# W3 times the last weights, moved out of its own stage and into the heads of attention

## The reference

```
attn_out = softmax(mask(q @ k.T / 8)) @ v       # mask: query and key have the same 6 sign bits
x  = attn_out as 1536 x 512
h  = x @ moe_w_in                               # 512 x 2048
y  = (s * relu(h)**2 + b) @ moe_w_out           # 2048 x 512
out = ((y @ w1) * (y @ w2)) @ w3 @ w_out        # 512 x 1024 (twice), 1024 x 1024, 1024 x 512
```

## Time and profile before

| | us |
|---|---|
| median of 3 runs (lowest, highest) | 792.26 (791.89, 794.51) |
| the profiled execution | 792.57 |
| its span, first to last instruction | 790.8 |
| PE busy | 763.3 (97%) |
| DVE busy | 458.7 (58%) |
| ACT busy | 369.1 (47%) |
| POOL busy | 238.9 (30%) |

### The profile page before, as it was taken

The page is one execution under the profiler, slowest core; times in us unless marked ns, Lnnn a source line. Parts: engine busy times, 40 slices in busy tenths (PEclk is TensorE's granted clock), DMA queues, the critical chain, the costliest instruction groups (busy, mean ns, idle before and its releaser), DMA issues.

```text
span 790.8 us, 11231 instructions
## 1 busy us (share of the span) xinstructions
PE 763.3 (97%) x3680; PEld 624.4 (79%) x3680; DVE 458.7 (58%) x809; ACT 369.1 (47%) x686; POOL 238.9 (30%) x150
## 2 busy tenths in 40 slices
PE   3999999999989899999999999999999999999998
PEld 2788888788878688888888888888887888888886
DVE  4899999999979711376665566655584201210220
ACT  2889998898889932443223132331352111211211
POOL 3347655674565744652022020220211000000000
PEclk9999999999999999999999999999999999999999
DMA  5343344334522232241011010110010010001001
GB/s 151 80 118 77 94 98 98 75 93 96 125 86 64 66 114 82 80 158 53 1 54 34 20 53 0 53 28 26 11 44 0 1 40 14 1 15 39 0 0 53
DMA packets 17680, 45.37 MB, mean 57 GB/s; under 512 B 4946, under 2 KB 6994, under 8 KB 17650
## 3 DMA queue, kind: packets, MB, share of 16 engines
q1 hardware_dynamic: 17650, 44.99, 20.7%
HBM read 37.75 MB, written 3.19 MB: 52 GB/s over the span
## 4 chain that ended last, share of the span: by engine, by line
PE 82%; DVE 7%; ACT 4%; issue 4%; DMA 2%; SPq 0%; POOL 0%; DVEq 0%; ACTq 0%
PE psum L986 55%; PE psum L1073 8%; PE psum L940 6%; PE psum L927 5%; PE psum L916 3%; DVE top L745 3%; PE psum L910 2%; ACT prob L524 2%; ACT pt_hi L540 1%; DVE pt_lo L759 1%; DVE x_lo L863 1%; PE psum L901 1%; DMA stage<-in_w_out 1%; PE psum L898 1%; DVE qm L738 1%
## 5 line engine op out<-in xcount | busy, mean ns | idle before, releaser
L759 DVE TENSOR_TENSOR pt_lo<-psum,pt_hi 128x384 fp32r<-128x384 f32 x192 | 97.8, 549 | 11.8 <-ACT pt_hi L540 10.2
L524 ACT ACTIVATE prob<-psum,exp_at 128x768 f32<-128x768 f32 x96 | 96.3, 1003 | 11.6 <-DVE exp_at L752 11.3
L745 DVE TENSOR_REDUCE top<-psum 128x1 f32<-128x768 f32 x96 | 90.9, 946 | 4.3 <-PE psum L916 4.1
L540 ACT ACTIVATE pt_hi<-psum 128x384 fp32r<-128x384 f32 x192 | 84.2, 493 | 19.1 <-PE psum L927 17.7
L632 ACT ACTIVATE relu<-psum 128x512 f32<-128x512 f32 x48 | 28.5, 596 | 137.0 <-PE psum L986 137.0
L986 PE MATMUL psum<-x_hi,w_b 128*128 128x512 f32 (+1 forms) x288 | 90.6, 396 | 0.0
L986 PE MATMUL psum<-x_hi,w_c 128*128 128x512 f32 (+1 forms) x288 | 90.6, 396 | 0.0
L927 PE MATMUL psum<-ident,prob 128*128 128x128 f32 x576 | 83.5, 280 | 4.2 <-DVE pt_lo L759 3.9
L886 DVE TENSOR_TENSOR ab<-psum,a_sb 128x512 f32<-128x512 f32 x24 | 16.6, 691 | 121.3 <-ACT a_sb L682 121.3
L840 DVE SCALAR_TENSOR_TENSOR relu<-psum,relu 128x512 f32<-128x512 f32 x48 | 33.1, 689 | 88.0 <-ACT relu L632 82.9
L403 POOL TENSOR_TENSOR w_b<-stage,w_b 128x1024 fp32r<-128x1024 f32 x18 | 43.6, 2425 | 125.0 <-ACT w_b L551 124.2
(11 more groups left out here) (91 smaller groups left out, 1459.7 us busy)
## 6 DMA issues: line engine op xcount, KB each, us to landing
raw<-in_qk SPq DMA_DIRECT2D x30, 384.0 KB, 5.2
stage<-in_w_out SPq DMA_DIRECT2D x12, 512.0 KB, 3.3
stage<-in_w3t SPq DMA_DIRECT2D x8, 512.0 KB, 3.9
stage<-in_w_in SPq DMA_DIRECT2D x8, 512.0 KB, 3.3
stage<-in_w SPq DMA_DIRECT2D x8, 512.0 KB, 3.2
raw_v<-in_v SPq DMA_DIRECT2D x16, 192.0 KB, 2.8
qm<-both_hi SPq DMA_DIRECT2D x16, 192.0 KB, 2.7
r_sb<-r_rows SPq DMA_DIRECT2D x16, 192.0 KB, 5.4
```

The lines of the kernel that those rows point to most:

```text
L524: act.activation(prob[:, t % 3], score[t % 2], ACT.Exp, bias=exp_at[:, t % 2, 1:2], scale=exp_at[:, t % 2, 0:1], accum_out=rsum[:, (t // 6 ...
L540: act.activation(pt_hi[:, u % 2, 3 * part:3 * part + 3, (t % 3) * P:(t % 3 + 1) * P], turned[part].rearrange("p (j q) -> p j q", j=3), ACT ...
L745: dve.tensor_reduce(top[:, t % 2, 1:2], score[t % 2], AX.X, ALU.max, negate=True).then_inc(top_done, 1)
L759: dve.tensor_tensor(pt_lo[at], turned[part].rearrange("p (j q) -> p j q", j=3), pt_hi[at].bitcast(F32), ALU.subtract).then_inc(pt_lo_done, 1)
```

## The change

The 8 blocks of `wc` are cut in halves of 256 columns (`g` = 0 to 15). Halves 0 to 13 are computed in heads 2 to 15, one per head, 6 matmuls in each of the head's last four tiles, into bank 7 after the head's sign bits are read from it; the last block is computed whole after attention. ACT copies each half to `wc_raw`, unsplit, and it is split into `wc_hi` (ACT) and `wc_lo` (POOL instead of DVE) in the first steps of the first layer. To have the weights in time, the last weights are loaded and split in pair 0, one chunk of W3 in every pair, and chunk 12 (the first layer's first) in pair 7. `x_raw` becomes a full-size buffer that shares its place with `x_lo`, and `wc_raw` one with `wc_lo`. PE, ACT and POOL write the middle pairs out instead of looping; DVE keeps its loop.

SP, the order of the loads:

```diff
+            for w in range(2):
+                load_w(w, w, w_out2[:, w * WCH:(w + 1) * WCH])
+
+            def pair(pr, first=False, last=False):
                 for k in range(2):
...
+                    if first and k == 0:
+                        load_w(2, 0, w_out2[:, 2 * WCH:3 * WCH])
+                    if first and k == 1:
+                        load_w(W3, 0, w3t[0])
+                    if not first and k == 0:
+                        load_w(W3 + pr, pr % 2, w3t[pr])
+                    if last and k == 0:
+                        load_w(of_layer(0), 0, w_in[0])
                     if last and k == 1:
-                        load_w(W3 + 1, 1, w3t[1])
+                        load_w(of_layer(0) + 1, 1, w_out[0])
                     sums_out(h, k, pr)
...
+                    if first and k == 0:
+                        load_w(3, 1, w_out2[:, 3 * WCH:4 * WCH])
                     sums_in(h, k, pr)
```

POOL, in the pairs (in pair 0 `w_out2_low(0)` stands first, 1 behind `scale_q`, 2 behind `k_lo`, 3 behind `x_of(0)`), and behind attention:

```diff
+            def w3_low(i):
+                w_low(W3 + i, high(w_b, i % 2), low(w_b, i % 2), i % 2)
+                pool.wait_ge(w_lo_done, W3 + i + 1)
...
                 if last:
-                    w_out2_low(2)
-                    w_out2_low(3)
+                    w3_low(pr)
...
                     k_lo(2 * pr + 3, 1)
                     pool.wait_ge(k_lo_done, 2 * pr + 4)
+                    w3_low(pr)
+                else:
+                    w_low(of_layer(0), high(w_c, 0), low(w_c, 0), 0)
+                    pool.wait_ge(w_lo_done, of_layer(0) + 1)
...
-            with pool.Fori(1, FT // 2) as ip:
-                for k in range(2):
-                    w_low(2 * ip + k + W3, high(w_b, k), low(w_b, k), k)
...
-            first_layer_weights(of_layer(0), 0)
+            w_low(of_layer(0) + 1, high(w_c, 1), low(w_c, 1), 1)
             pool.wait_ge(w_lo_done, of_layer(0) + 2)
             pool.memset(y_acc[:, :, :], 0.0).then_inc(y_zero, 1)
...
             for k in range(4):
                 w_low(W12_A + k, high(w_a, k), low(w_a, k), k % 2)
+            for i in range(FT):
+                pool.wait_ge(wc_hi_done, i + 1)
+                pool.tensor_tensor(wc_lo[:, i], wc_raw[:, i], wc_hi[:, i].bitcast(F32),
+                                   ALU.subtract).then_inc(wc_lo_done, 1)
```

ACT, at the end of a tile, after attention, and in steps 2 and 3 of the first layer:

```diff
+            def wc_copy(g):
+
+                act.wait_ge(wc_mm_done, g + 1)
+                act.activation(wc_raw[:, g // 2, (g % 2) * FC:(g % 2 + 1) * FC], wc_ps,
+                               ACT.Copy).then_inc(wc_raw_done, 1)
...
+                    if first and t in (1, 2, 5, 8):
+                        w = (1, 2, 5, 8).index(t)
+                        w_high(w, w // 2 + 1, w % 2, high(w_a, w))
+                    if (first and t == 11) or (last and t == 2) or (not (first or last) and t == 8):
+                        w_high(W3 + pr, (W3 + pr) // 2 + 1, pr % 2, high(w_b, pr % 2))
+                    if last and t == 8:
+
+                        act.wait_ge(k_lo_done, HEADS)
+                        w_high(of_layer(0), of_layer(0) // 2 + 1, 0, high(w_c, 0))
+                    if t % 6 == 5 and not first:
+                        wc_copy(h - 2)
...
+            act.wait_ge(wc_mm_done, HEADS - 1)
+            act.activation(wc_raw[:, FT - 1], psum[:, 2, :], ACT.Copy).then_inc(wc_raw_done, 1)
...
+            w_high(of_layer(0) + 1, of_layer(0) // 2 + 1, 1, high(w_c, 1))
...
+                    if first and k in (2, 3):
+                        for i in range(4 * k - 8, 4 * k - 4):
+                            wc_high(i)
```

PE, between `scores` (or `dots`) and `weighted`, and after attention; on DVE the loop that made `wc_lo` is gone:

```diff
+            def fused_terms(i, cols):
+                k = i % 2
+                return [(w[k][:, j], o[:, j, cols]) for j in range(FT)
+                        for w, o in ((w3_hi, wo2_lo), (w3_lo, wo2_hi), (w3_hi, wo2_hi))]
+
+            def fused_part(g, part, bits):
+
+                if part == 0:
+                    pe.wait_ge(w_lo_done, W3 + g // 2 + 1)
+                    pe.wait_ge(bits_done, bits)
+                    after(pe, wc_raw_done, g)
+                terms = fused_terms(g // 2, slice((g % 2) * FC, (g % 2 + 1) * FC))
+                for i in range(6 * part, 6 * part + 6):
+                    mm = pe.matmul(wc_ps, terms[i][0], terms[i][1], start=(i == 0), stop=(i == len(terms) - 1))
+                if part == 3:
+                    mm.then_inc(wc_mm_done, 1)
...
+                            after(pe, wc_raw_done, h - 2)
...
+                    if not first and t % 6 > 1:
+                        fused_part(h - 2, t % 6 - 2, min(2 * h + 4, 2 * HEADS))
...
-            for k in range(2):
-                fused(k, k)
-            with pe.Fori(1, FT // 2) as ip:
-                for k in range(2):
-
-                    pe.wait_ge(wc_lo_done, 2 * ip + k - 1)
-                    fused(2 * ip + k, k)
-
+            pe.wait_ge(w_lo_done, W3 + FT)
+            product(2, fused_terms(FT - 1, slice(0, DM))).then_inc(wc_mm_done, 1)
```

More of the change, by code:

```diff
@@ L57, in attention_mlp @@
         w_b = sb("w_b", [P, 4 * WCH], FR)
+        with ExitStack() as before_split:
+            wc_raw = sb("wc_raw", [P, FT, DM], F32, before_split)
+        wc_lo = sb("wc_lo", [P, FT, DM], FR)
         with ExitStack() as a:
@@ L289, in rows_of_chunk @@
                 return w[bass.ds(c, 1)].rearrange("o p n -> (o p) n")
-            pair(0)
-            for pr in range(1, PAIRS - 2):
+            pair(0, first=True)
+            for pr in range(1, PAIRS - 1):
                 pair(pr)
-            for w in range(2):
-                load_w(w, w, w_out2[:, w * WCH:(w + 1) * WCH])
-            for k in range(2):
[L297 to L303, removed]
-            pair(PAIRS - 1, last=True)
-            with sp.Fori(1, FT // 2) as ip:
-                for k in range(2):
[L307 to L310, removed]
+            pair(PAIRS - 1, last=True)
+            load_w(of_layer(1), 0, w_in[1])
+            load_w(of_layer(1) + 1, 1, w_out[1])
             for k in range(4):
@@ L414, in w_out2_low, with pair @@
                 pool.wait_ge(w_lo_done, w + 1)
-            def pair(pr, first=False, last=False, before_last=False):
+            def w3_low(i):
+                w_low(W3 + i, high(w_b, i % 2), low(w_b, i % 2), i % 2)
+                pool.wait_ge(w_lo_done, W3 + i + 1)
+            def pair(pr, first=False, last=False):
+                if first:
+                    w_out2_low(0)
                 if not first:
@@ L427, in pair @@
                     pool.wait_ge(q_scaled, 2 * pr + 4)
+                if first:
+                    w_out2_low(1)
                 if not first:
@@ L438, in pair @@
                     pool.wait_ge(k_lo_done, 2 * pr + 3)
+                if first:
+                    w_out2_low(2)
                 if not first:
@@ L446, in pair @@
                 pool.wait_ge(x_done, 4 * pr + 1)
-                if before_last:
-                    w_out2_low(1)
-                if not (last or before_last):
+                if first:
+                    w_out2_low(3)
+                if 2 * pr + 4 < HEADS:
                     scale_q(pr + 2, 0)
@@ L465, in _ @@
             pair(0, first=True)
-            with pool.Fori(1, PAIRS - 2) as pr:
+            for pr in range(1, PAIRS - 1):
                 pair(pr)
-            pair(PAIRS - 2, before_last=True)
             pair(PAIRS - 1, last=True)
-            w_low(W3 + 1, high(w_b, 1), low(w_b, 1), 1)
-            pool.wait_ge(w_lo_done, W3 + 2)
             x_of(2 * HEADS - 2, 2, PAIRS - 1)
@@ L562, in _, with pair @@
             exps(1, 1, 0)
-            def pair(pr, first=False, before_last=False, last=False):
+            def pair(pr, first=False, last=False):
                 for t in range(12):
@@ L584, in pair @@
                         v_high(2 * pr + 1, pr, 1)
[L585 to L592, removed]
-                        w_high(W3 + k, 3, k, high(w_b, k))
+                    if first and t in (1, 2, 5, 8):
[8 more added lines that the diff above has]
+                        wc_copy(h - 2)
             pair(0, first=True)
-            with act.Fori(1, PAIRS - 2) as pr:
+            for pr in range(1, PAIRS - 1):
                 pair(pr)
-            pair(PAIRS - 2, before_last=True)
             pair(PAIRS - 1, last=True)
@@ L622, in first_layer_weights, with wc_high @@
                     w_high(w + k, count, k, high(layer_buf[par], k))
-            first_layer_weights(of_layer(0), of_layer(0) // 2 + 1, 0)
-            fused(FT - 1, 1)
+            def wc_high(i):
+                act.activation(wc_hi[:, i], wc_raw[:, i], ACT.Copy).then_inc(wc_hi_done, 1)
             def hidden(n, k):
@@ L976, in _ @@
             pair(0, first=True)
-            with pe.Fori(1, PAIRS - 1) as pr:
+            for pr in range(1, PAIRS - 1):
                 pair(pr)
@@ L1077, in _ @@
             pe.wait_ge(w_lo_done, W12_A + 4)
+            pe.wait_ge(wc_lo_done, FT)
             pe.wait_ge(y_lo_done, KT)
```

54 lines of the change are left out of this document (12 added, 42 removed).

## The result

| | before | after |
|---|---|---|
| median of the runs | 792.94 us (791.89 to 794.51, 6 runs) | 787.38 us (785.65 to 790.35, 6 runs) |
| profiled execution, its span | 792.57, 790.8 us | 785.65, 783.7 us |
| ratio after / before | | 0.9934 (0.9915 to 0.9952) |

The change makes the kernel faster by 5.6 us. The forecast was 782.0, a gain of 10.6 us: the direction is right and the time lies inside the range, but only half of the gain came. So the question for the experiments was where the other 5 us went.

The account below looks back on a forecast made before the run. PE was taken to bound both attention, where it is held up only 1.2 us per head, and the wc stage; +25.6 us in attention and -36.2 behind it gave -10.6 on 792.57, so 782.0 us, range 773 to 791.

Parts of the forecast that it names:

- pairs 1 to 5: Ten heads of attention, 17.7 us each with the added matmuls: 177.0 for 157.0, +20.0 us.
- pair 6: Attention: loads of the last weights leave the pair, removing ACT's 2.45 us wait; 35.4 for 35.55, -0.15 us.
- head 14: First head of the last pair: 15.89 us becomes 17.6, +1.7 us.
- head 15: Last head: PE waits in its last three tiles, only one of four parts falls before; +0.5 us (0 to 2.9).
- pair 0: Start of attention: five added chunk copies on ACT and a possibly late chunk, +3.5 us (zero to 7.7).
- behind attention: From attention's end to the first product of out_of_hidden(0): 54.8 becomes 18.6 us, -36.2, with PE waiting 1.5 for the clearing.
- The price of the added matmul: Attention: each added matmul of 256 columns costs PE 0.120 us, 24 per head cost 2.9 us.
- Rival 3: Attention: weight load of the short matmul shows, 0.175 us each, +17.2 us, 799; chance 0.08.
- a quarter of today's 1.2 us survive as jitter: Attention: PE's work of 17.4 us per head plus part of today's hold-up gives 17.7 us per head.
- Rival 1: Attention: gaps around dots and the loops' register waits shrink too, 17.1 us per head, -7.8, near 774; chance 0.15.
- Rival 2: Attention: uneven copies on ACT delay turn, 18.6 us per head, +11.7, near 794, no change; chance 0.12.
- rival 4: Attention: W3's chunks come late, about 4 us in each of seven pairs, 810 us; chance 0.04.

Follow-up runs that it names:

- everything in time: Kernel after with W3's last chunk loaded in pair 6, y_acc cleared first, chunk 2 issued earlier, w_out2_low(3) behind k_lo: 776.69 us, 0.9805 of before.
- the mended kernel: Kernel after with only the load of W3's last chunk moved from pair 7 to the second half of pair 6: 783.81 us, 0.9883 of before.
- both edits and the later copies in pair 0: Kernel after with W3's last chunk loaded in pair 6, y_acc cleared first, last weights' chunks 2 and 3 copied at tiles 7 and 9: 781.44 us.

## Why the forecast was right in direction and wrong in size

| term | forecast | measured in the profiled execution |
|---|---|---|
| pairs 1 to 5 | +20.0 | +16.9 (173.9 for 157.0) |
| pair 6 | -0.15 | -0.9 (34.67 for 35.55) |
| head 14 | +1.7 | +4.4 (20.33 for 15.89) |
| head 15 | +0.5 | +2.8 (23.68 for 20.88) |
| pair 0 | +3.5 | +5.0 (tile 12 at 53.85 for 48.81) |
| behind attention | -36.2 | -35.5 (19.3 for 54.8) |
| sum | -10.6 | -7.2 (span -7.1, profiled time -6.9) |

- **The price of the added matmul held.** 0.120 us taken, 0.72 / 6 = 0.120 found. Rival 3 is out. The Trainium skill's rule in "TensorE: Matmul & The Clock Gate", section "The mechanism" (loads overlap matmuls only when the row groups differ), by which it would be an estimated 0.21 us as the prediction works out, is contradicted by these rows: all six matmuls have loads of 128 rows and 128 columns, and follow at 0.120.
- **The head was priced 0.4 us too high.** "I let a quarter of today's 1.2 us survive as jitter": none did. 17.33 us is PE's 14.5 + 2.9 to 0.1 us, PE never idle in the chain. Over the ten heads of pairs 1 to 5 this made the forecast 3.1 us too slow. Rival 1 (17.1 us) was a little closer for a head than the forecast, but its mechanism isn't seen: the period is the sum of the tiles as they stood, and writing out the loops brings nothing. Rival 2, the loop of copies, would have made it 18.6 us and doesn't occur.
- **The step that failed: heads 14 and 15, by the dismissal of rival 4.** The prediction said "Each chunk is issued behind two waits of SP and wanted at tile 8", so "four tiles, 11 us, lie between". That holds for pairs 1 to 6, where the copy starts 12.3 us behind the issue (72.69 to 85.00 in pair 1, 246.01 to 258.34 in pair 6). In the last pair the code wants the chunk at tile 2: 275.8 us, one microsecond after its issue. The mechanism of rival 4 was there at one pair of seven, with just its price ("about 4 us"): head 14 and 15 together +7.2 where +2.2 stood. Taking the chunk forward gives 4.2 of these 5 us back in the profile and 2.7 in the median. The rest lies in head 15, which takes 22.49 us without the stop: +1.6 where +0.5 stood, inside the bounds of that term.
- **Pair 0: the mechanism right, the size too small.** The prediction feared a chunk that is late as in pair 6 and took the middle. It came: the late one was the third chunk, not the first (5.5 us from issue to ACT), and cost PE 2.63 us. The sentence on POOL ("`w_out2_low` is also put ahead of `scale_q` and `q_lo` ...: nothing") gives no cover for the end of the pair: PE waits 0.96 us at the first `dots` of pair 1, and 4.04 us once it is ahead by the other edits. The idle time of POOL that was cited lies before `scale_q` of the pair's start, not before `k_lo` at its end. In the kernel after itself the wait is no loss of time, since the late chunk of W3 holds the same tile as long (4.72 us with and without it); it lies behind tile 12 and so isn't part of the +5.0.
- **Behind attention: right to 0.7 us.** The clearing is what comes late, as forecast; PE stands 2.29 instead of 1.5 us, and the rows put the difference down to the copy of `wc` on ACT, which goes ahead of the copy of chunk 13; the prediction has that start as soon as `x_lo` is done. No run changes this order alone.
- **The median against the profiled execution.** The prediction left out a difference of 0.3 us. In the kernel after the median is 1.7 us above the profiled run, which was the fastest of six, and the slower runs have the lower clock (785.65 at 0.998, 788.49 at 0.993, 790.35 at 0.989). The stops of PE and the low clock vanish together in everything in time (1.000 in ten of ten runs), but not the whole spread: its times still lie 2.8 us apart. This is the rest: 10.6 forecast, 6.9 in the profile, 5.6 in the median.

What the change is worth once the long stops are mended on both sides is 790.52 - 776.69 = 13.8 us, more than was forecast. The last measured version, everything in time, beats both kernels by 16.4 to 17 us and 10 us. What stays open is the late first chunk of W3 at the end of pair 0 (0.9 us), why the times spread at a clock of 1.000, and how the last 3.4 us divide.

## What to carry to other kernels

When transfers are spread over a loop, check each round by the code, the last and the first above all: the distance from issue to use that holds in the middle (twelve microseconds here) was one microsecond in the last round. A chunk that came 2.5 to 2.9 us late in the queue of a helper engine cost the bounding engine 2.1 to 2.6 us here, and in some executions 1 to 1.6 more while its clock was low; so mend the stops together and judge them together, for a stop that is left can hide what another edit won. And where the engine that a change loads becomes the only bound, as here, its own work is the period: an allowance for jitter of 0.3 us per head was 0.3 too much.

## What the hardware showed

- **A stop of PE of some 2 us or more can be followed by the low clock.** In the kernel after, PE stood for 2.50 us before 280.91, and its granted clock between 280 and 285 us was 0.66; the matmuls of 384 columns followed at 0.32 us up to 282.32 and at 0.175 from 285.13 on, the first being the 1.2 GHz level and the second the 2.4 GHz one. The tile with the stop took 6.36 us for 3.41 in the mended kernel; 2.50 of the 2.95 us between them are the stop. The five tiles behind it, which make the last part of attention, took 13.85 us in the profile of the kernel after run again and 12.46 in the mended one. It doesn't happen each time, and the length of the stop alone doesn't decide it: 2.63 us at 43.18 in the kernel after left the clock at 1.00 between 40 and 60, while 1.99 us at the same place gave 0.91 with W3's chunk early; before `out_of_hidden(0)`, 2.29 us left it at 1.00 in the one and gave 0.91 in the other. With both edits and the later copies in pair 0, it shows behind the stop of 4.04 us (columns as before):

```profile
60.00:80.00 20.00, 20.00 (x120) 17.78 (x119) 14.15 (x29) 13.72 (x29) 10.70 (x7) 0.88 0.44 109
```

- **A 512 KB load took longer right behind other loads.** The median is 3.5 us from issue to landing (3.3 in the earlier trace rows); the one issued in pair 0 at 35.35, behind a copy of queries (34.15) and a load of `v` (34.72), 192 KB each, was there at 40.9, after 5.5 us. Issued ahead of those two, at 31.01 in the kernel with everything in time, the same load took 3.5 us. The one issued at 40.57 in the kernel after, behind two loads of 384 KB (39.39), took 6.3 us.
